# Fillers at chunk 3, a bank-wise wait, norms, turns and folds placed anew, and outputs stored by tile

## The chip, the cores and the metric

The kernel runs on one core of one Trainium2 chip. The metric is the device time of one execution in microseconds; lower is better. Before the change the median of three runs is 759.34 us (758.0 to 760.5).

## The reference

Three blocks follow each other on 4 batches of 768 tokens. In NumPy, cut to what is computed:

```python
# 1. gated linear attention, 8 heads of 48, q k v alpha: (4, 8, 768, 48)
for t in range(S):
    state = alpha[:, :, t, :, None] * state + einsum('bhd,bhe->bhde', k[:, :, t], v[:, :, t])
    y[:, :, t] = einsum('bhd,bhde->bhe', q[:, :, t], state)
x = y by token: (4, 768, 384)
# 2. spatial gating
h = gelu_tanh(x @ w_in); u, v = halves of h            # w_in: 384 x 1024
v_n = (v - mean) / sqrt(var + 1e-6) * g_ln
v_s = einsum('ts,bsd->btd', w_sg, v_n) + b_sg          # w_sg: 768 x 768
x = x + (u * v_s) @ w_out                              # w_out: 512 x 384
# 3. Fourier mixing and a two-layer network
u = x + real(fft(fft(x, axis=1), axis=2))
un = (u - mean) / sqrt(var + 1e-6)
return u + maximum(un @ w_ch1, 0) @ w_ch2              # 384 x 1536, 1536 x 384
```

## The kernel before

Every fp32 product of blocks 2 and 3 is made of three passes over operands split into a high and a low fp32r part (`product`, L1115). ScalarE copies the high part (x_hi, gated_hi, hidden_hi, ut_hi, fold_hi, w_c_hi), and VectorE subtracts it to get the low part. So nearly every step of TensorE waits for a copy on ScalarE and a subtraction on VectorE. Each engine runs its steps in order, and the orders are lists written out by hand.

**The first batch's attention** is worked in six chunks of 128 tokens by `FIRST_PE`, `FIRST_DVE` and `FIRST_ACT`. VectorE's step "query" makes qu (qu_b for odd chunks), TensorE's step "scores" first transposes the decayed keys (L1136), then multiplies them with qu (L1146). `keep_warm` (L1121) issues small products on constants into a free bank; `WARM_SCORES` and `WARM_OUT` say at which chunks, how many.

**Phase 1** (block 2, and the next batch's attention beside it) runs once for each batch by `P1_ORDER`: products v0 to v5 and u0 to u7, each followed by a gelu on ScalarE, then s0 to s7, the spatial products with w_sg. s_i writes bank i % 2; u3 used bank 0 and u4 bank 1 before it. Behind the product of s_i come the output products o_(i-1) with w_out (L1115 too), and o7 at ("end", 0). VectorE and ScalarE make gated, gated_hi and gated_lo of each s_i; `add_x` adds the residual (x1_half), POOL copies two columns, and SP stores x1 to DRAM (x_scratch).

In the last batch's phase 1 the Fourier mixing of batch 0 is worked in: `LAST_P1_AT` lists, by the step they follow, fold 0 to 3 (VectorE), folded 0 and 1 (fold_hi and fold_lo), z 0 to 3 and nyquist (TensorE and copies), mix, stats, norm 0 to 5 (VectorE), turn 0 to 5 (TensorE transposes a normed tile, L1320) and turned 0 to 5 (ut_hi on ScalarE, ut_lo on VectorE). "split n" splits weight piece n of the second network; "split hi" and "split lo" are its halves. SP loads the pieces 6 to 11 as their buffers come free: piece 9 when s7 is done (s_done), 10 when gated 7 is done, 11 when o7 is done (po_done).

**Phase 2** (block 3) has 26 slots for a batch. Slot k holds h_k (hidden tile k: TensorE, relu on ScalarE, hidden_lo on VectorE), then o_(k-2) (output products into three accumulators), and then what a table says: `P2_FIRST_AT` for batch 0, `P2_AT` for the others, mixing the next batch. "left" steps are those of batch 0's own mixing that phase 1 left over. "keep" copies u into ub on ScalarE and waits for the last x1 store, since ub lies over x1's tile. h_k waits for hidden_lo k-2, o_k for hidden_lo k. "fin" adds the accumulators to ub after o11 and o23, and SP stores each tile. A fold reads x_quarters, of which SP loads half and POOL the other half by indirect DMA, with `kept` at 2 and turn 5 done as the condition for batch 1; u_new, the residual, is loaded by both queues in the same way.

## Time and profile before

| what | value |
|---|---|
| median of 3 runs | 759.34 us |
| profiled execution | 764.03 us |
| its span, first to last instruction | 762.2 us |
| TensorE, VectorE, ScalarE, POOL busy | 740.7, 460.4, 194.7, 74.6 us |
| mean granted TensorE clock | 0.983 |
| bytes moved by DMA | 54.04 MB |

Times in the rows are microseconds from the start of the span. PE is TensorE, PEld its weight load, DVE VectorE, ACT ScalarE, and SPq the DMA issues of SyncE. A bracket at the end of a timeline row is the idle time of that engine before the instruction, and what ended it. A granted clock of 1.00 is 2.4 GHz, 0.50 is 1.2 GHz.

### The profile page before, as it was taken

What the parts mean: (1) busy time and instruction counts of PE and PEld (TensorE: products, weight loads), DVE (VectorE), ACT (ScalarE), POOL (GpSimd) and SP (SyncE); (2) the same over time, 40 slices, a digit from 0 to 9 for tenths busy, and PEclk for the clock granted to TensorE, in tenths of its full rate; (3) what the DMA queues carried; (4) which work ended last, traced back from release to release, by engine and by line L of the source; (5) the groups of instructions that cost most, each with busy time, mean ns of one, the idle gap of its engine ahead of it and who ended that gap; (6) DMA issues with size and microseconds to landing.
All of it is one profiled execution on the core that took longest, in us unless ns stands there. A gap on an engine that the chain in (4) does not pass through costs nothing.

```text
span 762.2 us, 11949 instructions
## 1 busy us (share of the span) xinstructions
PE 740.7 (97%) x4824; PEld 717.4 (94%) x4824; DVE 460.4 (60%) x872; ACT 194.7 (26%) x366; POOL 74.6 (10%) x122
## 2 busy tenths in 40 slices
PE   8999999999999999999998889999999999999997
PEld 7889999999999999988998879999999999999997
DVE  7979858797666966668588455445353735432221
ACT  1236111242112411134314322213211332122111
POOL 1013000030000300042110302001210010000000
PEclk9799999999999999999999989999999999999999
DMA  9623132231321313062315402002120020000000
GB/s 294 180 56 121 48 94 79 79 94 47 95 79 42 84 48 94 32 187 85 105 57 171 136 1 85 21 32 63 37 68 1 31 62 31 0 31 1 1 32 31
DMA packets 21000, 54.04 MB, mean 71 GB/s; under 512 B 2356, under 2 KB 14776, under 8 KB 20952
## 3 DMA queue, kind: packets, MB, share of 16 engines
q1 hardware_dynamic: 18104, 44.53, 19.3%
q0 software_dynamic: 2704, 8.71, 3.9%
q8 instruction: 34, 0.56, 0.3%
q10 hardware_dynamic: 144, 0.13, 0.1%
q14 instruction: 14, 0.11, 0.1%
HBM read 43.90 MB, written 9.46 MB: 70 GB/s over the span
## 4 chain that ended last, share of the span: by engine, by line
PE 88%; DVE 6%; issue 2%; ACT 2%; DMA 1%; POOL 1%; DVEq 0%; SPq 0%
PE bank L1115 72%; PE bank L1173 5%; PE bank L1146 3%; PE bank L1169 3%; PE bank L1161 2%; PE bank L1204 1%; PE bank L1136 1%; PE bank L1320 1%; DVE u_kept L1075 1%; DMA x_quarters<-x_scratch,mirrored_rows 1%; DMA decay_k_q<-in_akq 1%; DVE fold_f_sin L988 0%; POOL x_quarters L623 0%; ACT vn_hi L707 0%; ACT w_c_hi L694 0%
## 5 line engine op out<-in xcount | busy, mean ns | idle before, releaser
L1115 PE MATMUL bank<-ut_hi,w_c 128*128 128x384 f32 x576 | 164.7, 341 | 1.9 <-DVE hidden_lo L1066 1.9
L1066 DVE SCALAR_TENSOR_TENSOR hidden_lo<-bank,hidden_hi 128x384 fp32r<-128x384 f32 x96 | 53.4, 556 | 126.9 <-ACT hidden_hi L795 125.5
L1115 PEld LDWEIGHTS bank<-ut_hi,w_c 128*128 128x128 f32 x576 | 106.3, 189 | 2.3 <-DVE hidden_lo L1066 2.3
L795 ACT ACTIVATE hidden_hi<-bank 128x384 fp32r<-128x384 f32 x96 | 47.3, 492 | 205.4 <-PE bank L1115 205.4
L1115 PE MATMUL bank<-w_c_hi,hidden_hi 128*128 128x384 f32 x288 | 96.7, 336 | 0.7 <-DVE u_kept L1075 0.7
L1115 PE MATMUL bank<-ut_lo,w_c 128*128 128x384 f32 x288 | 96.9, 336 | 0.0
L1115 PE MATMUL bank<-w_c_hi,hidden_lo 128*128 128x384 f32 x288 | 96.3, 334 | 0.0
L1115 PE MATMUL bank<-w_c_lo,hidden_hi 128*128 128x384 f32 x288 | 96.2, 334 | 0.0
L1115 PE MATMUL bank<-w_sg_hi,vn_hi 128*128 128x384 f32 x192 | 67.6, 352 | 1.8 <-ACT u_gelu L728 1.8
L1115 PE MATMUL bank<-w_sg_lo,vn_hi 128*128 128x384 f32 x192 | 65.2, 340 | 0.0
L1115 PE MATMUL bank<-w_sg_hi,vn_lo 128*128 128x384 f32 x192 | 65.1, 339 | 0.0
L1115 PEld LDWEIGHTS bank<-w_c_hi,hidden_hi 128*128 128x128 f32 x288 | 54.2, 188 | 1.9 <-issue 1.9
L1115 PEld LDWEIGHTS bank<-ut_lo,w_c 128*128 128x128 f32 x288 | 54.6, 190 | 0.0
L1115 PEld LDWEIGHTS bank<-w_c_lo,hidden_hi 128*128 128x128 f32 x288 | 54.2, 188 | 0.0
L1115 PEld LDWEIGHTS bank<-w_c_hi,hidden_lo 128*128 128x128 f32 x288 | 54.1, 188 | 0.0
L749 ACT CAST gated_hi<-gated 128x384 fp32r<-128x384 f32 x32 | 16.4, 512 | 141.6 <-DVE gated L973 141.6
L1115 PEld LDWEIGHTS bank<-w_sg_hi,vn_hi 128*128 128x128 f32 x192 | 36.8, 192 | 3.5 <-issue 2.4
L1173 PE MATMUL bank<-values,sm 128*128 128x48 f32 x288 | 39.9, 266 | 0.0
L969 DVE SCALAR_TENSOR_TENSOR gated<-bank,g_col,bias_sg 128x384 f32<-128x384 f32 x32 | 19.7, 615 | 30.3 <-PE bank L1115 30.2
L1173 PEld LDWEIGHTS bank<-values,sm 128*128 128x128 f32 x288 | 37.2, 192 | 0.0
L889 DVE TENSOR_TENSOR sm<-bank,constants 128x512 f32<-128x512 f32 x42 | 27.0, 685 | 16.7 <-PE bank L1146 16.7
L1115 PEld LDWEIGHTS bank<-w_sg_lo,vn_hi 128*128 128x128 f32 x192 | 37.0, 193 | 0.0
(191 smaller groups left out, 1466.7 us busy)
## 6 DMA issues: line engine op xcount, KB each, us to landing
decay_k_q<-in_akq SPq DMA_DIRECT2D x19, 673.8 KB, 5.3
x_scratch<-x_half SPq DMA_DIRECT2D x8, 579.0 KB, 3.9
out_tiles<-u_kept SPq DMA_DIRECT2D x24, 192.0 KB, 2.0
values<-in_v SPq DMA_DIRECT2D x18, 192.0 KB, 5.1
x_quarters<-x_scratch SPq DMA_DIRECT2D x16, 168.9 KB, 3.4
raw_first_a<-in_w_first SPq DMA_DIRECT2D x3, 768.0 KB, 4.4
raw_first_b<-in_w_first SPq DMA_DIRECT2D x3, 768.0 KB, 4.7
raw_weights_b<-in_w_second SPq DMA_DIRECT2D x3, 768.0 KB, 4.3
```

The source lines that it names most:

```text
L749: nc.scalar.copy(gs[0][:, i % 3, :], gt[:, i % 3, :]).then_inc(ghi_done, 1)
L795: nc.scalar.activation(hid[0][:, i % 4, :], HB[i % 2][:, 0:HS], ACT.Relu).then_inc(hhi_done, 1)
L889: nc.vector.tensor_tensor(sm[:, :, x, :], sc[x][:].rearrange("p (a t) -> p a t", a=4), mask[:].unsqueeze(1).to_broadcast([P, 4, P]), ALU.m ...
L969: nc.vector.scalar_tensor_tensor(out=gt[:, i % 3, :], in0=GB[i % 2][:, 0:HS], scalar=g_col[:, f:f + 1], in1=bias_sg[:, h * HS:(h + 1) * HS ...
L1066: nc.vector.scalar_tensor_tensor(out=hid[1][:, i % 4, :], in0=HB[i % 2][:, 0:HS], scalar=0.0, in1=f32(hid[0][:, i % 4, :]), op0=ALU.max, o ...
L1075: nc.vector.tensor_tensor(ub[:, HT * i + j, :], ACC[j][:, 0:DM], ub[:, HT * i + j, :], ALU.add).then_inc(fin_done, 1)
L1115: ins = nc.tensor.matmul(dst, a, c, start=start and n == 0, stop=stop and n == len(passes) - 1)
L1136: ins = nc.tensor.transpose(ky[:, g * PR:(g + 1) * PR], kd[:, g, :], ident[0:PR, 0:PR])
L1146: ins = nc.tensor.matmul(sc[j][:, g * P:(g + 1) * P], kd[at, g, :], qu[at, g, :], start=True, stop=True)
L1161: ins = nc.tensor.matmul(sc[0][0:PR, g * PP:(g + 1) * PP], kn[:, g, :], values[:, g * PP:(g + 1) * PP], start=True, stop=True)
L1169: nc.tensor.matmul(ky[:, g * PP:(g + 1) * PP], qu[:, g, :], std[:, c % 2, g, :], start=True, stop=False, skip_group_check=True)
L1173: ins = nc.tensor.matmul(ky[:, h * D:(h + 1) * D], sm[:, g, j, :], values[:, h * D:(h + 1) * D], start=c == 0, stop=True, skip_group_check ...
```

## The change

- `WARM_SCORES` gets five filler products at chunk 3's scores.
- In phase 1, s0 waits for the gelu of u3 and s1 for that of u4 (in place of all eight at s0); o0 waits for all eight. In batch 0 the old wait stays.
- In the last phase 1, "folded 0" moves from behind u5 to behind u7. A new place, "product of s" 7, lies between s7's product and what follows it; turn 2 and turned 2 move there. Norm 3 moves up behind s6, turn 3 and norms 4 and 5 behind s7, turns 4 and 5 to the end of the phase. The split of piece 8 stands whole behind s7, and the high half of piece 9 at the end of the phase.
- In the first phase 2 only turned 3, 4 and 5 are left over. keep 0 and keep 1 both stand in slot 2. The folds move from slots 5 to 7 to slots 6 to 9, z from 8 to 10 to 10 to 12, mix 0 from 10 to 13, and the steps behind it by one to three slots. Pieces 9, 10 and 11 are split at h0, h3 and h4 (before: h0, h1, h3).
- SP loads piece 11 ahead of the last x1 store, and waits for POOL's quarters of batch 1 before it loads that batch's residual.
- In the last batch, o22 and o23 are worked together, accumulator by accumulator, with a semaphore of their own, and the last additions wait for it tile by tile.

```diff
 
 
-WARM_EARLY, WARM_SCORES, WARM_OUT = 8, {0: 3}, {0: 5, 1: 4}
+WARM_EARLY, WARM_SCORES, WARM_OUT = 8, {0: 3, 3: 5}, {0: 5, 1: 4}
 
...
          19: [("turn", 2), ("turned", 1), ("norm", 3)], 20: [("turned", 2), ("turn", 3), ("norm", 4)],
          21: [("turn", 4), ("norm", 5)], 22: [("turn", 5)], 24: [("turned", 3), ("turned", 4)], 25: [("turned", 5)]}
-P2_FIRST_AT = {0: [("left", ("turn", 3)), ("left", ("norm", 4)), ("left", ("turned", 3))],
-               1: [("left", ("turn", 4)), ("left", ("norm", 5)), ("left", ("turned", 4))],
-               2: [("left", ("turn", 5)), ("left", ("turned", 5)), ("keep", 0)], 3: [("keep", 1)],
-               5: [("fold", 0)], 6: [("fold", 1), ("fold", 2)], 7: [("fold", 3), ("folded", 0)],
-               8: [("folded", 1), ("z", 0)], 9: [("z", 1), ("z", 2)], 10: [("z", 3), ("nyquist", 0), ("mix", 0)]}
+P2_FIRST_AT = {1: [("left", ("turned", 3)), ("left", ("turned", 4))], 2: [("left", ("turned", 5)), ("keep", 0), ("keep", 1)],
+               6: [("fold", 0)], 7: [("fold", 1)], 8: [("fold", 2)], 9: [("fold", 3), ("folded", 0)],
+               10: [("folded", 1), ("z", 0)], 11: [("z", 1), ("z", 2)], 12: [("z", 3), ("nyquist", 0)], 13: [("mix", 0)],
+               14: [("stats", 0)], 15: [("mix", 1)], 16: [("stats", 1), ("mix", 2)], 17: [("stats", 2)],
+               18: [("norm", 0)], 19: [("turn", 0), ("norm", 1)], 20: [("turn", 1), ("turned", 0), ("norm", 2)],
+               21: [("turn", 2), ("turned", 1), ("norm", 3)], 22: [("turned", 2), ("turn", 3), ("norm", 4)],
+               23: [("turn", 4), ("norm", 5)], 24: [("turn", 5), ("turned", 3), ("turned", 4)], 25: [("turned", 5)]}
 
...
 
 P2_ORDER = phase2_order(P2_AT)
-P2_FIRST = phase2_order({k: P2_FIRST_AT.get(k, [] if k < 11 else P2_AT.get(k, [])) for k in range(2 * NF + LAG)})
+P2_FIRST = phase2_order(P2_FIRST_AT)
 FOURIER_STEPS = ("fold", "folded", "z", "nyquist", "mix", "stats", "norm", "turn", "turned")
-SPLIT_IN_P2 = {0: 9, 1: 10, 3: 11}
+SPLIT_IN_P2 = {0: ("split lo", 9), 3: ("split", 10), 4: ("split", 11)}
 
 
 LAST_P1_AT = {("v", 5): [("fold", 0)], ("u", 3): [("fold", 1), ("fold", 2)], ("u", 4): [("fold", 3)],
-              ("u", 5): [("folded", 0)], ("s", 0): [("folded", 1), ("z", 0), ("z", 1), ("split", 6)],
+              ("u", 7): [("folded", 0)], ("s", 0): [("folded", 1), ("z", 0), ("z", 1), ("split", 6)],
               ("s", 1): [("z", 2), ("z", 3), ("nyquist", 0)], ("s", 2): [("split", 7), ("mix", 0), ("stats", 0)],
               ("s", 3): [("mix", 1), ("stats", 1)], ("s", 4): [("mix", 2)],
               ("s", 5): [("stats", 2), ("norm", 0), ("norm", 1)],
-              ("s", 6): [("turn", 0), ("turn", 1), ("turned", 0), ("norm", 2), ("turned", 1), ("split hi", 8)],
-              ("s", 7): [("turn", 2), ("turned", 2), ("split lo", 8)], ("end", 0): [("norm", 3)]}
+              ("s", 6): [("turn", 0), ("turn", 1), ("turned", 0), ("norm", 2), ("turned", 1), ("norm", 3)],
+              ("product of s", 7): [("turn", 2), ("turned", 2)],
+              ("s", 7): [("turn", 3), ("norm", 4), ("norm", 5), ("split", 8)],
+              ("end", 0): [("turn", 4), ("turn", 5), ("split hi", 9)]}
 
...
         hlo_done = sem("hlo_done")
         o_done = sem("o_done")
+        o_tile_done = sem("o_tile_done")
         fin_done = sem("fin_done")
...
                     sp.wait_ge(z_done, 4)
                 need(sp, kept, 2 * m)
+                if m == 1:
+                    sp.wait_ge(quarters_in[1], 128)
                 sp.dma_start(ua[:, 0:HT, 0:DM], x1_dram[m][0:HS, 0:DM].rearrange("(j p) n -> p j n", p=P)).then_inc(
...
             sp.wait_ge(gt_done, 8 * B)
             load_piece(sp, NP1 + KD + 1)
-            store_x1(B - 1, "end", 0)
             sp.wait_ge(po_done, 8 * B)
             load_piece(sp, NP1 + KD + 2)
+            store_x1(B - 1, "end", 0)
             load_quarters(1)
...
                             vn_hi(b, NT - 4 + i)
                     elif step == "s":
+                        if isinstance(b, int) and b == B - 1:
+                            beside_last_phase1("product of s", i)
                         act.wait_ge(gt_done, 8 * b + i + 1)
...
                         need(act, o_done, k - 3)
                         nc.scalar.activation(hid[0][:, i % 4, :], HB[i % 2][:, 0:HS], ACT.Relu).then_inc(hhi_done, 1)
-                        if i in SPLIT_IN_P2 and isinstance(b, int) and b == 0:
-                            split_hi(SPLIT_IN_P2[i])
+                        if i in SPLIT_IN_P2 and isinstance(b, int) and b == 0 and SPLIT_IN_P2[i][0] == "split":
+                            split_hi(SPLIT_IN_P2[i][1])
 
...
                         nc.vector.tensor_tensor(gt[:, i % 3, :], gt[:, i % 3, :], ug[:, f, h * HS:(h + 1) * HS],
                                                 ALU.mult).then_inc(gt_done, 1)
+                        if isinstance(b, int) and b == B - 1:
+                            beside_last_phase1("product of s", i)
                         gated_lo(b, i)
...
                                                        op1=ALU.subtract).then_inc(hlo_done, 1)
                         if i in SPLIT_IN_P2 and isinstance(b, int) and b == 0:
-                            split_lo(SPLIT_IN_P2[i])
+                            split_lo(SPLIT_IN_P2[i][1])
                     elif step == "fin":
                         dve.wait_ge(kept, 2 * b + i + 1)
-                        dve.wait_ge(o_done, 2 * NF * b + NF * (i + 1))
+                        last = isinstance(b, int) and b == B - 1 and i == 1
+                        if not last:
+                            dve.wait_ge(o_done, 2 * NF * b + NF * (i + 1))
                         for j in range(HT):
+                            if last:
+                                dve.wait_ge(o_tile_done, j + 1)
                             nc.vector.tensor_tensor(ub[:, HT * i + j, :], ACC[j][:, 0:DM], ub[:, HT * i + j, :],
...
                             if i == 0:
                                 pe.wait_ge(vlo_done, NT * (b + 1))
-                                pe.wait_ge(ug_done, 8 * (b + 1))
                                 if isinstance(b, int) and b == 0:
+                                    pe.wait_ge(ug_done, 8)
                                     pe.wait_ge(w_lo_done, NP1)
+                            if i < 2:
+                                pe.wait_ge(ug_done, 8 * b + 4 + i)
                             if i >= 2:
...
                                       [w[:, t, h * HS:(h + 1) * HS] for w in w_sg]) for t in range(NT)]
                                     ).then_inc(s_done, 1)
+                            if isinstance(b, int) and b == B - 1:
+                                for what, n in LAST_P1_AT.get(("product of s", i), []):
+                                    mixing(0, what, n)
 
...
                             f = j % 4
                             pe.wait_ge(glo_done, 8 * b + j + 1)
+                            if j == 0:
+                                pe.wait_ge(ug_done, 8 * (b + 1))
                             if j == 4:
...
                         if f == 0:
                             need(pe, fin_done, NT * b + HT * h)
+                        if isinstance(b, int) and b == B - 1 and i >= 2 * NF - 2:
+                            if i == 2 * NF - 1:
+                                for j in range(HT):
+                                    product(ACC[j][:, 0:DM],
+                                            [([x[:, n % 4, j * P:(j + 1) * P] for x in hid],
+                                              [w[:, n % NF, :] for w in w_c2]) for n in (i - 1, i)],
+                                            start=False).then_inc(o_tile_done, 1)
+                            continue
                         for j in range(HT):
```

## Rows read from the trace of the kernel before

**Rows 1.** The page of the profile: TensorE's line of the busy times

```profile
PE 740.7 (97%) x4824; PEld 717.4 (94%) x4824; DVE 460.4 (60%) x872; ACT 194.7 (26%) x366; POOL 74.6 (10%) x122
```

**Rows 2.** Waits of TensorE: us in total, times, longest us

```profile
PE bank L1115 <- DVE fold_lo L1001: 3.5, 1, 3.5
PE bank L1115 <- ACT u_gelu L728: 2.0, 2, 1.8
PE bank L1320 <- DVE u_norm_early L1048: 2.0, 2, 1.5
PE bank L1115 <- DVE hidden_lo L1066: 1.9, 1, 1.9
PE bank L1146 <- DVE qu_b L875: 1.8, 1, 1.8
...
PE bank L1115 <- DVE gated_lo L915: 0.7, 1, 0.7
...
PE bank L1115 <- DVE z_lo L1007: 0.6, 1, 0.6
```

**Rows 3.** Windows: length, busy PE, PEld, DVE, ACT, POOL, granted clock, DMA, GB/s

```profile
26.85:36.95 10.10, 10.10 (x44) 9.44 (x44) 9.94 (x15) 1.44 (x3) 0.00 (x0) 0.50 0.49 158
...
108.60:111.95 3.35, 3.35 (x22) 3.12 (x21) 1.29 (x2) 0.36 (x1) 0.00 (x0) 0.50 0.80 229
361.20:364.55 3.35, 3.35 (x13) 3.35 (x12) 0.00 (x0) 0.00 (x0) 0.00 (x0) 0.50 0.02 5
443.25:449.85 6.60, 5.32 (x22) 5.32 (x23) 3.12 (x5) 1.42 (x3) 0.00 (x0) 0.50 0.00 0
```

**Rows 4.** Timeline around chunk 3: start us, us, engine, line, instruction, idle before

```profile
9.95 1.38 PE L1121 MATMUL bank<-constants 128*128 128x128 f32 x10
...
24.48 0.69 DVE L875 TENSOR_TENSOR qu_b<-decay_k_q_d,fwd_b 112x512 f32<-112x512 f32 x1
...
37.21 0.69 DVE L875 TENSOR_TENSOR qu<-decay_k_q,fwd 112x512 f32<-112x512 f32 x1
...
41.62 1.16 PE L1146 MATMUL bank<-qu,kd 48*128 48x128 f32 x16
```

**Rows 5.** Timeline ahead of the last batch's first spatial product

```profile
353.24 1.46 DVE L910 TENSOR_TENSOR vn_lo<-v_gelu,vn_hi 128x512 fp32r<-128x512 f32 x2
...
358.35 0.83 ACT L757 CAST fold_hi<-fold_f_cos 97x772 fp32r<-97x772 f32 x1 [2.69 <-DVE fold_f_cos L997]
...
359.09 0.87 ACT L728 ACTIVATE u_gelu<-bank 128x384 f32<-128x384 f32 x2
```

**Rows 6.** Timeline at the seam, then two of the DMA issue rows (landing last)

```profile
404.49 0.55 DVE L1053 TENSOR_TENSOR ut_lo<-bank,ut_hi 128x384 fp32r<-128x384 f32 x1
...
405.97 0.34 SPq L480 DMA_DIRECT2D raw_weights_a<-in_w_second  x1
...
412.50 0.38 SPq L499 DMA_DIRECT2D x_scratch<-x_half  x1
...
x_scratch<-x_half SPq DMA_DIRECT2D x8, 579.0 KB, 3.9
...
raw_weights_a<-in_w_second SPq DMA_DIRECT2D x1, 768.0 KB, 4.2
```

**Rows 7.** Timeline of the quarters, a weight split and the first fold

```profile
423.58 1.76 DVE L839 TENSOR_TENSOR w_c_lo<-raw_weights_d,w_c_hi 128x1536 fp32r<-128x1536 f32 x1 [0.81 <-ACT w_c_hi L694]
...
424.88 1.35 POOL L623 DMA_INDIRECT x_quarters<-x_scratch,mirrored_rows  x1 [12.41 <-ACT u_kept L789]
...
429.01 0.92 POOL L623 DMA_INDIRECT x_quarters<-x_scratch,mirrored_rows  x1 [0.30 <-issue]
...
435.35 1.77 DVE L988 TENSOR_TENSOR fold_f_cos<-x_quarters 97x1544 f32<-97x1544 f32 x1 [6.33 <-DMA x_quarters<-x_scratch,mirrored_rows]
```

**Rows 8.** Timeline at the end of the kernel

```profile
754.02 0.56 DVE L1066 SCALAR_TENSOR_TENSOR hidden_lo<-bank,hidden_hi 128x384 fp32r<-128x384 f32 x1 [2.56 <-ACT hidden_hi L795]
...
758.25 1.49 DVE L1075 TENSOR_TENSOR u_kept<-bank,u_kept 128x384 f32<-128x384 f32 x3 [3.67 <-PE bank L1115]
```

## Prediction

> **What bounds the kernel now.** I read the page first: TensorE is busy for 740.7 of 762.2 us [rows 1], so an edit pays only where it removes one of TensorE's few waits or stretches at the half clock, and the whole of what can be had is small. The waits of TensorE come next [rows 2]: 3.5 us for a fold, 2.0 for u_gelu, 2.0 for two normed tiles, 1.9 for hidden_lo, 1.8 for qu_b, 0.7 for gated_lo, 0.6 for z_lo. They lie in three places (chunk 3 of the first batch, the start of the last spatial products, the seam of the two phases with what follows it). Then the windows in which the granted clock is 0.50, that is 1.2 and not 2.4 GHz [rows 3]: 10.1 us behind the wait for qu_b, 3.4 us from 108.6, 3.4 us behind the wait for u_gelu, and 6.6 us that begin inside the wait for the fold. A wait thus costs itself and, in three of the four long ones, half of a stretch behind it. The timeline around each place gives who is late [rows 4 to 8].
>
> **Fillers at chunk 3.** Five filler products are 10 instructions, 1.2 to 1.4 us as the 1.38 us of the same ten at 9.95 [rows 4]. They stand where TensorE waits 1.76 us for qu_b (ready at 25.17), so they cost nothing as long as they are shorter than that wait; at the half clock they would take 2.4 to 2.8 us and cost up to 1.0. About 0.5 us of idle stays. If the clock holds, the 10.1 us at 1.2 GHz shrink to some 5. VectorE doesn't follow: it is busy for 9.94 of these 10.10 us [rows 3] and finishes chunk 4's queries at 37.90 whatever TensorE does [rows 4]. Chunk 4's scores, which began at 41.62, can't begin before. Gain 41.6 - 38.0 = 3.6 us, not 5. Behind that point TensorE is full and VectorE had its own waits on TensorE, so both move up together. Bounds: 0 (the clock falls all the same) to 3.6. I take 3.6.
>
> **Bank-wise wait.** s0 now asks for u3's gelu, s1 for u4's, and only the first output product for all eight; in addition ScalarE copies the first fold behind u7 and not behind u5. Before, that copy at 358.35 held the last two gelus until 359.96 [rows 5]. What s0 needs else is v_lo, done at 354.70 [rows 5]. So s0 starts at once: 1.8 us of wait (2.0 in two waits, this the longest) [rows 2] and half of the 3.4 us behind it [rows 3] go, 3.5 together. The product after s0 is z0, which waits for folded_lo; VectorE ends that at about 361.1 and s0 takes 3.1 us (18 products; 9 are half a slot of 3.12, the 0.56 + 2.56 of [rows 8]) and ends at 361.2. That is the thinnest cover here: if it fails, 0.3 us.
>
> **Turns and norms at the seam.** Turns 3, 4 and 5 go from phase 2 to the end of phase 1. Norm 3 can follow turned 1, whose ut_lo ends at 405.04 [rows 6], so turn 3 is no longer behind three x1 additions (1.5 us, as the three of [rows 8]) and a weight split of 1.76 [rows 7]. I count from the end of s7 at 405.8, just before SP's issue at 405.97 that waits for it [rows 6]: turn 2 0.3, o6 1.56, turn 3 0.3, a wait for gated_lo of 0.4 (0.7 before, since ScalarE now copies gated 7 without the weight split ahead of it), o7, two turns 0.6, h0, h1, h2, o0 at 1.56 each: 416.8, where before the same work ended at 419.8. The waits gone are 2.0 for the two norms [rows 2] + 0.3 = 2.3 us; I take these and leave the rest. What is late next is piece 9, split at h0: issued at 405.97 and 4.2 us to landing [rows 6], copied by ScalarE until about 412.0, its low half by VectorE until 414.9, while o0 wants it at 415.2. One us more of landing costs 0.7. Bounds 1.0 to 3.0.
>
> **What the moved DMAs change.** On SP's queue the last x1 store goes behind piece 11, which waits for po_done: the store leaves at about 412.9, as before (412.50), but has 768 KB ahead of it. ScalarE's two keep copies wait for it, and both now stand in slot 2, ahead of the relu of h3. At 3.9 us to landing [rows 6] it is there at 416.8, and piece 11 beside it may make it 418.5. TensorE first misses that relu at h5, at 423.0; so the store may be 2 us later still before it costs anything. kept then reaches 2 near 419.8 against 424.6, and the quarter loads start 4.8 us earlier. On SP the residual of batch 1 now waits for POOL's quarters; behind it in that queue stands only the first half's output store, due some 40 us later.
>
> **Folds later.** The first fold waited 6.33 us for quarters, which landed 5.4 us after the last POOL issue had ended [rows 7], with the residual's 576 KB in the same engines. It held hidden_lo (1.9 us), then z0 waited 3.5 us for the fold, and the clock fell. Now the issues end near 425 and the quarters land by 430.4 at the same 5.4 us, sooner with the residual held back (427 to 431); the fold is asked for at 428.7 (slot 6 starts at 426.1, its h takes 1.56 and relu and hidden_lo the next 1.0), in slot 6, and the first product that would miss hidden_lo 7 is h9 at 435.4: a fold that starts by 433 is free. z0 comes in slot 10, behind one fold operation per slot (1.76 to 1.84 us of VectorE in 3.12). Gain 1.9 + 3.5, and half of the 5.32 us that TensorE worked in the slow window from 443.25 [rows 3], 2.7: 8.1. The product behind z3 is now in the next slot, 0.6 more. Bounds 4 (the landing as late as before in absolute time, a third of the stall and one slow stretch back) to 8.7.
>
> Here a rule speaks against the change. The first POOL issue took 1.35 us, the later ones 0.92, and it overlapped a weight split of 1.76 us, which ended at 425.34, by 0.46 [rows 7]. By the Trainium skill ("SBUF — State Buffer", Who interferes with whom) a VectorE instruction with two SBUF inputs blocks GpSimd's SBUF reads for its whole length; the rows agree (0.43 longer). Two splits of 1.76 us now run beside these POOL issues. By the rule they put the landing at 431 to 432 instead of 428, still inside the cover.
>
> **Output by tile.** The last two output steps run tile by tile. Three additions (1.49 us, 0.47 apart) followed the last product [rows 8]; now one does. Gain 0.95. Skipping o22 takes away what stood before o23, but hidden_lo 23 ends at 754.58 [rows 8] and o21 about 755.0, two half slots before the last product's end, so no wait comes.
>
> **Sum.** 3.6 + 3.5 + 2.3 + 8.1 + 0.6 + 0.95 = 19.1 us. The profiled execution took 764.03 us (span 762.2 and 1.8 around it), the median of the runs is 759.34, so 4.7 less. Taken from the profiled time the sum gives 744.9, from the median 740.2. Part of the 4.7 may be slow stretches that the change removes anyway. I take the middle, **742.5**.
>
> **The rivals.** (1) The fillers don't hold the clock, because the products behind them are small: in the window from 108.6 the clock fell after an idle time of only 0.7 us. Then 3.6 is missing: 746. (2) Quarters, store or piece 9 land late and a new stall at slots 2 to 7 takes the place of the fold's: 3 to 5 us back, 746 to 749. For it: the DMA engines are full around these transfers; against: covers of 2 and 4 us. (3) The edits do nothing that a run shows, since each freed wait is given back to VectorE, 60% busy over all but nearly full at chunk 3 and at the seam: 758. Against: it waits for TensorE in between. (4) Slower: ScalarE stands at keep 0 until the x1 store behind piece 11 lands; each us past 420.5 stalls TensorE from h5 on one for one, and moves kept and the quarters. It decides from the 19 us that the rest gains: only a landing 29 us after the issue makes 762. The landing of these stores is 3.9 us [rows 6], so little speaks for it.
>
> **How the numbers follow.** Forecast 0.64, rival 1 0.15, rival 2 0.14, rival 3 0.04, rival 4 0.03. The range runs from 740.2 less the 1.7 us that the slow window from 108.6 costs (it may shift away), 738.5, to rival 2's 749. About 0.3%, 2.3 us, is what a measurement of this kernel can tell from no change. Faster 0.94 (the forecast, rivals 1 and 2, and a quarter of rival 3), same 0.03 (the rest of rival 3), slower 0.03 (rival 4).
>
> **What would show it.** In the profile of the changed kernel: ten filler instructions before chunk 3's scores and a granted clock of 1.00 from 27 to 37; chunk 4's scores at 38; no wait for u_gelu before the last batch's s0; turns 3 to 5 ahead of h0, o0 without a wait; the first fold not waiting for quarters or less than 4 us; no window at 0.50 in phase 2; one addition behind the last product. A busy time of TensorE near 732 (740.7 less the halves of three slow stretches, plus the fillers) and a span near 743 would be right. Wrong would be a granted clock of 0.50 behind the fillers, or a wait of TensorE for hidden_lo in slots 4 to 9.

## The result and the profile after

The changed kernel takes 741.49 us (median of 4 runs, 741.35 to 743.57); the kernel before, run beside it, 759.92 us (4 runs, 758.0 to 763.5). The ratio is 0.976, 95% interval 0.972 to 0.980: 18.4 us less, between the medians. The profiled execution took 741.35 us; the one of before was one of the slowest of its kernel, so the two traces stand 22.7 us apart, and what follows says which of the two differences is meant.

The page of the profile after: span, busy times, the row of the granted clock over 40 slices.

```profile
span 739.5 us, 11977 instructions
...
PE 730.5 (99%) x4834; PEld 709.3 (96%) x4834; DVE 460.0 (62%) x872; ACT 194.5 (26%) x366; POOL 76.8 (10%) x122
...
PEclk9999999999999999999999999999999999999999
```

TensorE is busy for 730.5 us, where [rows 1] had 740.7, and its clock is at 2.4 GHz in every slice. The waits of TensorE after (us in total, times, longest):

```profile
PE bank L1141 <- DVE state_decayed L1093: 1.7, 1, 1.7
PE bank L1130 <- DVE w_in_lo L848: 0.9, 1, 0.9
PE bank L1151 <- ACT y_by_token_odd L710: 0.7, 1, 0.7
PE bank L1161 <- DVE qu_b L884: 0.6, 1, 0.6
...
PE bank L1130 <- DVE gated_lo L924: 0.2, 1, 0.2
```

Of the seven waits of [rows 2] the ones for the fold, u_gelu, the norms, hidden_lo and z_lo are gone; qu_b fell from 1.8 to 0.6 and gated_lo from 0.7 to 0.2. One is new: the wait for w_in_lo behind chunk 3, which the trace of before, with TensorE at half clock there, does not have. The windows after that answer to [rows 3] (length, busy PE, PEld, DVE, ACT, POOL, granted clock, DMA, GB/s):

```profile
24.00:37.00 13.00, 11.49 (x100) 10.56 (x100) 12.73 (x21) 3.84 (x5) 0.00 (x0) 1.00 0.50 152
100.00:110.00 10.00, 9.34 (x77) 8.98 (x76) 6.23 (x11) 1.08 (x3) 0.00 (x0) 1.00 0.33 89
352.00:362.00 10.00, 10.00 (x70) 9.81 (x69) 7.53 (x13) 4.74 (x7) 0.00 (x0) 1.00 0.08 33
430.00:450.00 20.00, 20.00 (x147) 19.92 (x146) 9.19 (x16) 5.14 (x11) 3.71 (x4) 1.00 0.16 39
```

All four are at 1.00. In the first VectorE is busy for 12.73 of 13.00 us while TensorE now has 1.5 us of idle: the bound there has passed to VectorE.

TensorE's timeline of after, at four places: the fillers with the scores of chunk 3 and of chunk 4; the first product of s0; the turns of the seam; the last product.

```profile
23.03 1.29 PE L1136 MATMUL bank<-constants 128*128 128x128 f32 x10
24.95 1.16 PE L1161 MATMUL bank<-qu_b,kd_b 48*128 48x128 f32 x16 [0.63 <-DVE qu_b L884]
...
37.68 1.16 PE L1161 MATMUL bank<-qu,kd 48*128 48x128 f32 x16
...
352.62 0.33 PE L1130 MATMUL bank<-w_sg_hi,vn_hi 128*128 128x384 f32 x1
...
396.80 0.49 PE L1342 MATMUL bank<-constants,u_norm_early 128*128 128x128 f32 x3
...
398.69 0.49 PE L1342 MATMUL bank<-constants,u_norm_early 128*128 128x128 f32 x3
399.40 0.45 PE L1130 MATMUL bank<-w_out_hi,gated_hi 128*128 128x384 f32 x1 [0.22 <-DVE gated_lo L924]
...
401.08 0.82 PE L1342 MATMUL bank<-constants,u_norm_early 128*128 128x128 f32 x6
...
736.22 0.34 PE L1130 MATMUL bank<-w_c_hi,hidden_lo 128*128 128x384 f32 x1
```

Chunk 4's scores begin at 37.68, where [rows 4] had 41.62. The place 352.62 of s0 was 360.10 before, and the end of s7, 396.80, was 405.8: 3.9, 7.5 and 9.0 us earlier. TensorE's last product, at 757.80 before, starts at 736.22, 21.6 us earlier, and the span is 22.7 us shorter. Over the whole span TensorE is idle for 21.5 us before (762.2 - 740.7) and for 9.0 after (739.5 - 730.5).

What carries the fold at the start of phase 2, from the timelines of SP, ScalarE, POOL and VectorE of after, one engine behind the other:

```profile
403.60 0.38 SPq L504 DMA_DIRECT2D x_scratch<-x_half  x1
...
409.31 2.21 ACT L798 COPY u_kept<-u_new_early 128x1152 f32<-128x1152 f32 x2 [1.81 <-DMA x_scratch<-x_half]
...
411.80 1.02 POOL L630 DMA_INDIRECT x_quarters<-x_scratch,mirrored_rows  x1 [8.23 <-ACT u_kept L798]
413.12 0.93 POOL L630 DMA_INDIRECT x_quarters<-x_scratch,mirrored_rows  x1 [0.31 <-issue]
414.36 1.50 POOL L630 DMA_INDIRECT x_quarters<-x_scratch,mirrored_rows  x1 [0.31 <-issue]
416.17 1.82 POOL L630 DMA_INDIRECT x_quarters<-x_scratch,mirrored_rows  x1 [0.30 <-issue]
...
413.31 1.76 DVE L848 TENSOR_TENSOR w_c_lo<-raw_weights_c,w_c_hi 128x1536 fp32r<-128x1536 f32 x1 [0.81 <-ACT w_c_hi L701]
...
415.45 1.75 DVE L848 TENSOR_TENSOR w_c_lo<-raw_weights_d,w_c_hi 128x1536 fp32r<-128x1536 f32 x1
...
420.15 1.77 DVE L999 TENSOR_TENSOR fold_f_cos<-x_quarters 97x1544 f32<-97x1544 f32 x1
```

The fold, which had waited 6.33 us for the quarters [rows 7], has no bracket: they are there when slot 6 asks, though with nothing to spare, since SP, which waits for POOL's quarters now, issues the residual at 420.13. The keep copies do wait, 1.81 us, for the store issued at 403.60, but TensorE doesn't follow.

### The profile page after: what moved, and what is told of

Its sections match the earlier page's. It is cut to its first block, busy times and chain, and to the rows that moved or that the text cites. A ratio compares the mean times of both kernels' runs of the same rounds, so it can differ in the third digit from the quotient of the medians.

```text
span 739.5 us, 11977 instructions
## 1 busy us (share of the span) xinstructions
PE 730.5 (99%) x4834; PEld 709.3 (96%) x4834; DVE 460.0 (62%) x872; ACT 194.5 (26%) x366; POOL 76.8 (10%) x122
## 4 chain that ended last, share of the span: by engine, by line
PE 94%; DVE 4%; issue 1%; DMA 1%; ACT 0%; SPq 0%; DVEq 0%
PE bank L1130 79%; PE bank L1188 5%; PE bank L1161 3%; PE bank L1184 2%; PE bank L1176 2%; PE bank L1151 1%; PE bank L1342 1%; PE bank L1219 1%; DVE u_kept L1090 1%; DMA decay_k_q<-in_akq 1%; DVE fwd_b L880 0%; DVE fwd L880 0%; DVE rev_b L868 0%; DVE w_in_lo L848 0%; DVE sm L898 0%
## 5 line engine op out<-in xcount | busy, mean ns | idle before, releaser
L1130 PE MATMUL bank<-ut_hi,w_c 128*128 128x384 f32 x576 | 162.8, 339 | 0.0
L1130 PEld LDWEIGHTS bank<-w_sg_hi,vn_lo 128*128 128x128 f32 x192 | 36.0, 188 | 0.0
```

The costliest lines, as they stand in the source:

```text
L1130: ins = nc.tensor.matmul(dst, a, c, start=start and n == 0, stop=stop and n == len(passes) - 1)
```

## The experiments

Each kernel was timed beside the kernel before on the same chip. Before ran 48 times in these comparisons: 756.2 to 765.1 us, with a mean granted clock of 0.983 to 0.995, never 1.000. They were taken in three groups, each on a chip of its own. That spread decides what single edits can show, so it comes first. Before's runs by clock (mean time, runs): 0.983: 764.0 (12); 0.984: 764.5 (4); 0.986: 762.3 (4); 0.988: 760.8 (7); 0.990: 759.3 (7); 0.992: 757.9 (4); 0.993: 757.8 (1); 0.995: 757.4 (9). A straight line through all 48 is, rounded, time = 753.9 us + 600 us x (1 - clock), and the runs scatter about it by 0.8 us. A clock of 0.983 is 25.8 us at 1.2 GHz in 760, so a microsecond of half clock costs about 0.4 us of time. With this line each run can be read at full clock (its time less 600 x (1 - clock)), which takes out of the comparison how the clock happened to fall. The mean of each kernel so read, with twice its standard error:

| kernel | runs | median us | mean clock | read at full clock |
|---|---|---|---|---|
| before | 48 | 760.2, 760.2, 761.3 in the three groups | 0.988 | 753.9 ± 0.2 |
| before + fillers | 10 | 758.71 | 0.993 | 754.3 ± 0.6 |
| before + tile outputs | 10 | 762.46 | 0.987 | 753.6 ± 0.2 |
| before + bank-wise wait | 10 | 757.75 | 0.991 | 751.7 ± 0.5 |
| before + later folds | 9 | 754.13 | 0.991 | 747.7 ± 0.8 |
| after with the old seam | 4 | 744.66 | 0.999 | 744.5 ± 0.3 |
| after with the old fold slots | 4 | 746.81 | 0.998 | 745.7 ± 0.6 |
| after without the fillers | 4 | 742.11 | 0.997 | 741.4 ± 0.3 |
| after | 4 | 741.49 | 0.999 | 741.5 ± 0.6 |

The slope is that of before; for kernels at a clock of 0.999 it hardly matters. For before it does: none of its runs is above 0.995, so its 753.9 is an extrapolation, and its groups do not lie exactly on the line (0.5 us above it at 0.995, 0.8 below at 0.992, 1.0 above at 0.984). The ± in the table is the scatter alone; differences between the kernels of before and those of after can be off by about 1 us more, an estimate from these distances.

**The fillers, added alone and taken out alone.** To before:

```diff
-WARM_EARLY, WARM_SCORES, WARM_OUT = 8, {0: 3}, {0: 5, 1: 4}
+WARM_EARLY, WARM_SCORES, WARM_OUT = 8, {0: 3, 3: 5}, {0: 5, 1: 4}
```

> The kernel before with the five filler products at chunk 3's scores and nothing else. Theory (the wait for qu_b lets the clock fall, the fillers hold it, and VectorE limits what that gives): granted clock 1.00 from 27 to 37 us, chunk 4's scores near 37.7 in place of 41.62, and 3.6 to 3.9 us less, 755.5 to 756.5; if the window at the half clock near 108 goes with it, 1.7 more. Rival (the products behind the fillers are too small to hold the clock): a window at 0.50 between 27 and 37 stays, gain under 1.5 us. Rival (the gain is the full half of the 10.1 us): 5 us less.

Measured: 758.71 us (757.38 to 760.29), ratio 0.9964, interval 0.9933 to 0.9994. Windows of its profiled execution:

```profile
26.85:36.95 10.10, 9.45 (x78) 8.49 (x74) 9.94 (x16) 2.02 (x4) 0.00 (x0) 1.00 0.58 181
108.00:115.00 7.00, 7.00 (x54) 7.00 (x54) 4.38 (x8) 0.60 (x2) 1.21 (x1) 1.00 0.21 55
356.50:360.00 3.50, 3.50 (x13) 3.50 (x12) 0.18 (x1) 0.00 (x0) 0.00 (x0) 0.51 0.02 5
441.00:446.00 5.00, 5.00 (x25) 5.00 (x24) 1.78 (x3) 1.00 (x2) 0.00 (x0) 0.66 0.01 3
```

The stretch that stood at 0.50 in [rows 3] is at 1.00; the one near 108 is gone too, and the ones of u_gelu and of the fold remain. The median moved by 1.4 us against the group's 760.15 and the mean by 2.0 (758.74 against 760.79), short of the 3.6 expected. The other way round, after with `3: 5` taken out:

> The changed kernel without the fillers at chunk 3. Theory: the half clock from 27 to 37 us comes back and with it 3.6 to 3.9 us, 745 to 745.5. If the slow window near 108 was tied to the shift of the schedule by the fillers, it comes back too: 747. Rival (the clock fell in the profile of before by chance of its phase): no change in most runs, 741.5.

Measured: 742.11 us (741.46 to 748.14), ratio 0.9755, interval 0.9682 to 0.9827: not to be told from after, as the rival had it. Two of the four runs have a clock of 1.000 without any filler (741.46 and 741.59), one has 0.988 (748.14). In the profiled one (742.62, clock 0.998) the wait for qu_b is 1.8 us again and the clock falls only briefly:

```profile
25.00:30.00 5.00, 4.23 (x31) 4.01 (x32) 4.46 (x7) 2.81 (x3) 0.00 (x0) 0.66 0.46 122
30.00:36.00 6.00, 6.00 (x47) 5.50 (x46) 5.88 (x10) 0.86 (x2) 0.00 (x0) 1.00 0.80 258
```

What the stretch costs can be read without the jitter of the start, as the distance from chunk 3's scores to chunk 4's. It is 12.73 us after (24.95 to 37.68) and in before + fillers (25.97 to 38.70); 16.39 in before (25.23 to 41.62) and in before + bank-wise wait (25.38 to 41.77), both with the clock down for about 10 us; 13.29 in after without fillers (25.77 to 39.06), with the clock down for 3.4 us. And it is 12.72 in before + later folds, which has no fillers and waited 1.76 us like before, but kept its clock. Its timeline, and then its window:

```profile
25.30 1.16 PE L1150 MATMUL bank<-qu_b,kd_b 48*128 48x128 f32 x16 [1.76 <-DVE qu_b L879]
...
38.02 1.16 PE L1150 MATMUL bank<-qu,kd 48*128 48x128 f32 x16
```

```profile
26.00:38.00 12.00, 11.12 (x96) 10.23 (x92) 11.81 (x18) 2.48 (x5) 0.00 (x0) 1.00 0.41 135
```

So the price of 3.66 us is right where the clock falls, but the fall behind this wait is not certain. Same wait and same work behind it gave about 10 us of half clock, 3.4 us, or none. Over all the profiled executions: without fillers at chunk 3 the clock falls there in four of five, with two or five fillers in none of nine.

**Fewer fillers, and fillers at a second place.** After with two products instead of five, and after with two more ahead of the wait for y_by_token_odd in the first piece of phase 1:

```diff
-WARM_EARLY, WARM_SCORES, WARM_OUT = 8, {0: 3, 3: 5}, {0: 5, 1: 4}
+WARM_EARLY, WARM_SCORES, WARM_OUT = 8, {0: 3, 3: 2}, {0: 5, 1: 4}
```

> The changed kernel with two fillers at chunk 3's scores and not five, so about 1.3 of 1.76 us of wait stay idle. Theory (the clock falls with the share of idle time, by chance of phase, and without fillers two of four runs fell): some runs of ten show a clock of 0.995 or less and take 744 to 748, the fastest 741.4 and the median 741.5 to 743. Rival (any work in the gap is enough): as the changed kernel with five.

```diff
+                    if not before and isinstance(n, int) and n == 1 and c == 3:
+                        keep_warm(sc[1], 2)
                     need(pe, yn_done, i - before)
```

> The changed kernel with two more filler products in the first phase 1, at batch 1's chunk 3, where TensorE waits 0.66 us for y_by_token_odd. They are 4 instructions, 0.5 us, inside that wait. Theory (what is left of the spread between the runs of the changed kernel, 741.4 to 745.6, is a stretch at half clock behind such small waits, by chance of phase): the fastest runs stay at 741.4, fewer runs show a clock under 0.999, and the median falls by 0 to 0.5 us. Rival (the rest of the spread comes from another place): the same spread as the changed kernel, 741.4 to 745.6.

Measured: 741.50 us (741.47 to 742.07, 6 runs) with two, 741.34 us (741.17 to 742.24, 6 runs) with a second place. All twelve runs have a clock of 1.000. With two products it is held although 1.3 us of the wait for qu_b stay, as the rival had it. The second place is 0.15 us under after, less than either kernel's own spread, so it is not shown to be a gain: with two products and no second place the six clocks are 1.000 as well.

**The bank-wise wait alone**, in before, with the copy of the fold behind u7 as in the change:

```diff
-              ("u", 5): [("folded", 0)],
+              ("u", 7): [("folded", 0)],
...
-                                pe.wait_ge(ug_done, 8 * (b + 1))
                                 if isinstance(b, int) and b == 0:
+                                    pe.wait_ge(ug_done, 8)
                                     pe.wait_ge(w_lo_done, NP1)
+                            if i < 2:
+                                pe.wait_ge(ug_done, 8 * b + 4 + i)
```

> The kernel before with the bank-wise waits of s0, s1 and o0 and the first folded step moved behind u7, nothing else. Theory: the 1.8 us wait for u_gelu ahead of the last batch's s0 goes and so does the 3.4 us at half clock behind it: 3.5 us less, 756. Rival (z0 or VectorE waits instead): the wait goes but under 1.5 us are won.

Measured: 757.75 us (752.25 to 760.05, 10 runs), ratio 0.9933, interval 0.9896 to 0.997. The wait of 1.8 us for u_gelu is gone from its list (one of 0.2 is left) and the clock is 1.00 behind it:

```profile
27.00:38.00 11.00, 11.00 (x50) 10.16 (x49) 10.81 (x16) 1.44 (x3) 0.00 (x0) 0.53 0.48 149
352.00:362.00 10.00, 10.00 (x69) 9.81 (x68) 8.94 (x13) 3.91 (x8) 0.00 (x0) 1.00 0.25 80
```

At full clock it stands 2.2 us under before; 1.8 was the wait. The median moved by 2.4 us and the mean by 3.9, where 3.5 was expected. One of its runs, at a clock of 1.000, took 752.25. In that profile TensorE's wait for the fold is 1.9 us, not 3.5, with the clock down around it (433 to 437, 440 to 444). TensorE, at half clock ahead of the wait, came to it about 1.7 us later, half of the 3.4, and so waited 1.6 us less: that stretch cost next to nothing.

**The copy of the fold, put back** behind u5 in after:

```diff
-              ("u", 7): [("folded", 0)],
+              ("u", 5): [("folded", 0)],
```

> The changed kernel with the first folded step back behind u5, the bank-wise waits kept. Theory (the waits of s0 and s1 need only u3 and u4, whose gelus come before that copy): s0 still starts at once; only o0 needs all eight gelus, 3 us later: no change, 741.5. Rival (the move of the copy was what freed s0): the wait ahead of s0 and a stretch at half clock come back, 743.5 to 745.

Measured: 743.78 us (741.57 to 745.64, 4 runs); the runs above 745 have a clock of 0.995, those at 0.999 and 1.000 took 741.57 and 742.35. In the profiled one (741.57) no wait for u_gelu stands ahead of s0. The bank-wise wait alone does it. Read at full clock the kernel stands at 742.0 ± 0.7, after at 741.5 ± 0.6; whether the copy's place has a part in the two lower clocks, four runs don't say.

**The folds: the later slots alone, and everything but them.** To before, from slot 6 on the table of after (slots 0 to 3 as before); and after with before's slots 5 to 10:

```diff
-               5: [("fold", 0)], 6: [("fold", 1), ("fold", 2)], 7: [("fold", 3), ("folded", 0)],
-               8: [("folded", 1), ("z", 0)], 9: [("z", 1), ("z", 2)], 10: [("z", 3), ("nyquist", 0), ("mix", 0)]}
+               6: [("fold", 0)], 7: [("fold", 1)], 8: [("fold", 2)], 9: [("fold", 3), ("folded", 0)],
+               10: [("folded", 1), ("z", 0)], 11: [("z", 1), ("z", 2)], 12: [("z", 3), ("nyquist", 0)], 13: [("mix", 0)],
...
```

> The kernel before with the folds, z, nyquist and mix of the first phase 2 in the later slots (folds 6 to 9, z 10 to 12, mix 0 at 13), nothing else; turns, keeps and DMA order as before. The quarters should land at 435.3 as before, the fold is asked for at 431.6, and the first product that misses hidden_lo 7 is h9 at 438.4. Theory (the slots give most of the cover): VectorE waits 3.7 in place of 6.3 us, TensorE waits for neither hidden_lo nor the fold at z0: 5.4 us of waits less and the window at half clock behind them gone in the profile, time 752 to 755. Rival (only the earlier quarters make the cover): TensorE still waits 2 us or more there, 757 or more.

> The changed kernel with the folds, z, nyquist and mix of the first phase 2 in the slots of before (folds 5 to 7, z 8 to 10), keeps, turns and DMA order as changed. Theory (both the earlier quarters and the later folds are needed): the quarters are in by 418 to 420, the fold is asked for at 416.5, so VectorE stands 2 to 3 us, folds in two slots of 3.12 us delay z0 by 1 to 3 us; 743 to 746 and perhaps one stretch at half clock. Rival (the earlier quarters alone did it): within 0.7 us of 741.5.

Measured: the slots alone 754.13 us (749.59 to 755.86, 9 runs), ratio 0.9899, interval 0.9865 to 0.9933; after without them 746.81 us (745.93 to 749.17, 4 runs), ratio 0.9836. In the first no wait for hidden_lo or z_lo is left, and one of 0.2 us for fold_lo, although the fold still waits 3.43 us for its quarters. In the second the quarters come at 420.8 and not at 435.3, but the fold is asked for earlier too and waits 2.50 us for them; TensorE waits 3.0 us for fold_lo and, as before, 0.6 for z_lo. The fold of the first; then VectorE from the step ahead of the fold to the low part that z0 needs, in the second; then TensorE's wait there:

```profile
430.43 1.77 DVE L992 TENSOR_TENSOR fold_f_cos<-x_quarters 97x1544 f32<-97x1544 f32 x1 [3.43 <-DMA x_quarters<-x_scratch,mirrored_rows]
```

```profile
417.75 0.55 DVE L1074 SCALAR_TENSOR_TENSOR hidden_lo<-bank,hidden_hi 128x384 fp32r<-128x384 f32 x1
420.80 1.77 DVE L996 TENSOR_TENSOR fold_f_cos<-x_quarters 97x1544 f32<-97x1544 f32 x1 [2.50 <-DMA x_quarters<-x_scratch,mirrored_rows]
...
428.96 0.95 DVE L1009 TENSOR_TENSOR fold_lo<-fold_f_cos,fold_hi 97x772 fp32r<-97x772 f32 x1
```

```profile
PE bank L1127 <- DVE fold_lo L1009: 3.0, 1, 3.0
```

The slots are worth 6.2 us on before and 4.2 us on after, both at full clock, where 743 to 746 had been expected for the second kernel. The lesser gain on after is what the earlier quarters had taken already (no wait for hidden_lo, half a microsecond less for the fold). What is left in the second is mostly the quarters after all: VectorE was free at 418.30 and stood for 2.50 us, then worked without a pause from 420.80 to 429.91, and z0 had been due at 427.0. Had the quarters been there at 418.3, the same work would have ended about 427.4, an estimate from these rows, and about 0.5 of the 3.0 us would be left. So the later slots alone are enough, and quarters another 2.5 us earlier would have done nearly as much; that no run tried.

**What brings the quarters early, undone.** After without SP's new wait for the quarters ahead of the residual, and after with the x1 store ahead of piece 11 again:

```diff
-                if m == 1:
-                    sp.wait_ge(quarters_in[1], 128)
```

> The changed kernel without SP's wait for POOL's quarters ahead of the residual load of batch 1. Theory: the residual's 576 KB share the DMA engines with the quarters as before, these land 1 to 3 us later, at 420 to 423, and the first fold has cover until about 425: no change of the time, 741.5, but VectorE may wait for quarters by up to 2 us. Rival (the hold is what keeps TensorE from waiting): 1 us or more slower.

```diff
+            store_x1(B - 1, "end", 0)
             sp.wait_ge(po_done, 8 * B)
             load_piece(sp, NP1 + KD + 2)
-            store_x1(B - 1, "end", 0)
```

> The changed kernel with SP's last x1 store again ahead of piece 11. Theory: the store leaves at the same time (403.6) with less traffic ahead of it and lands 1 to 2 us earlier, ScalarE's 1.81 us wait at the first keep shrinks, and as TensorE had cover there the time is the same, 741.5. Rival (the order of store and piece decides the time of the quarters and with it the fold): 1 us or more either way.

Measured: 741.66 us (741.52 to 744.68, 4 runs) and 741.84 us (741.22 to 743.71, 4 runs). The fold of the first, then the keep copies of the second:

```profile
422.39 1.77 DVE L997 TENSOR_TENSOR fold_f_cos<-x_quarters 97x1544 f32<-97x1544 f32 x1 [1.93 <-DMA x_quarters<-x_scratch,mirrored_rows]
```

```profile
408.56 2.21 ACT L798 COPY u_kept<-u_new_early 128x1152 f32<-128x1152 f32 x2 [0.28 <-DMA x_scratch<-x_half]
```

Without the hold the quarters come some 2 us later and VectorE waits 1.93 us for them. With the store first the keep copies start 0.75 us earlier, though the store left 0.78 us later in that execution, so 1.5 us sooner after its issue. Neither reaches TensorE, and neither shows in the time of four runs, in these slots.

**The seam, put back**: turns 3 to 5, the norms, the weight splits and keep 1 where before has them, the rest as after.

```diff
-              ("product of s", 7): [("turn", 2), ("turned", 2)],
-              ("s", 7): [("turn", 3), ("norm", 4), ("norm", 5), ("split", 8)],
-              ("end", 0): [("turn", 4), ("turn", 5), ("split hi", 9)]}
+              ("s", 7): [("turn", 2), ("turned", 2), ("split lo", 8)], ("end", 0): [("norm", 3)]}
...
-SPLIT_IN_P2 = {0: ("split lo", 9), 3: ("split", 10), 4: ("split", 11)}
+SPLIT_IN_P2 = {0: ("split", 9), 1: ("split", 10), 3: ("split", 11)}
```

> The changed kernel with turns 3 to 5, norms 3 to 5, the split of pieces 8 to 11 and keep 1 placed as before; later folds, DMA order, fillers, bank-wise waits and tile outputs stay. Theory: the two waits for norms at h1 and h2 (0.5 and 1.5 us) and the longer wait for gated_lo come back, 2.3 us, and the quarters start later by as much again without touching the fold: 743.5 to 744.5. Rival (the later quarters take the cover of the fold): 746 or more with a wait of TensorE for hidden_lo near slot 6.

Measured: 744.66 us (744.13 to 747.38, 4 runs), ratio 0.9804, interval 0.9752 to 0.9855. Its waits:

```profile
PE bank L1342 <- DVE u_norm_early L1059: 2.0, 2, 1.5
...
PE bank L1130 <- DVE gated_lo L924: 0.7, 1, 0.7
```

Both stalls are back, and profile against profile, both at a clock of 1.000, it is 744.13 - 741.35 = 2.8 us, as expected (743.5 to 744.5), and no wait for hidden_lo appears.

**The outputs by tile alone**, in before: the change's own lines for o_tile_done.

```diff
+                            if last:
+                                dve.wait_ge(o_tile_done, j + 1)
...
+                        if isinstance(b, int) and b == B - 1 and i >= 2 * NF - 2:
+                            if i == 2 * NF - 1:
```

> The kernel before with o22 and o23 of the last batch worked together, accumulator by accumulator, and the last three additions waiting tile by tile, nothing else. Theory: one addition and not three behind the last product, 0.95 us less, 758.8 to 759. Rival (skipping o22 exposes hidden_lo 23, or the store of the last tile queues behind the others): 0 to 0.4 us less or a wait of TensorE ahead of the last step.

Measured: 762.46 us (757.26 to 764.01, 10 runs), ratio 1.0006, interval 0.9972 to 1.004. The median shows nothing of it: read at full clock it is 0.3 us under before, give or take 0.3, where 0.95 was expected. The trace shows it: from the start of TensorE's last product to the end of the span it is 3.3 us here (756.82 to 760.1), 4.4 in before (757.80 to 762.2), 3.3 after (736.22 to 739.5). The end of after on VectorE:

```profile
734.59 0.56 DVE L1090 TENSOR_TENSOR u_kept<-bank,u_kept 128x384 f32<-128x384 f32 x1 [1.62 <-PE bank L1130]
735.55 0.56 DVE L1090 TENSOR_TENSOR u_kept<-bank,u_kept 128x384 f32<-128x384 f32 x1 [0.41 <-PE bank L1130]
736.60 0.56 DVE L1090 TENSOR_TENSOR u_kept<-bank,u_kept 128x384 f32<-128x384 f32 x1 [0.49 <-PE bank L1130]
```

Two additions run while TensorE still multiplies; in [rows 8] all three came behind it.

## Why the prediction was right, step by step

The forecast of 742.5 us is 1.0 us above the 741.49 measured; the sum of 19.1 us stands against 18.4 between the medians. That it came so near is in part luck: the forecast is the middle between 744.9 (from the profiled time) and 740.2 (from the median), and the prediction chose the middle with one sentence and no working. It helps to split that sum into waits and clock. The waits in it are 1.8 (u_gelu) + 2.3 (seam) + 5.4 and 0.6 (folds, z_lo) + 0.95 (outputs) = 11.05 us; the clock is 3.6 + 1.7 + 2.7 = 8.0. Measured at full clock, before and after are 753.9 - 741.5 = 12.4 us apart. The single edits add up to that: bank-wise wait 2.2, later folds 6.2, seam 2.9, outputs 0.3 by the runs and 1.1 by the trace, together 11.6 to 12.4, and so do the two traces, with 21.5 - 9.0 = 12.5 us less idle time of TensorE. The rest, 18.4 - 12.4 = 6.0 us, is the clock. So the waits were sized 1.3 us too small and the clock 2.0 us too large, and the two errors partly cancel. The split is good to about 1 us, as said under the table.

**Fillers.** The mechanism holds: they fit in the wait, 0.63 us of idle stays (0.5 forecast), and chunk 4's scores follow VectorE, at 37.68 (38 forecast). The step that was too sure is that the 3.6 us are there in every execution. On before they were worth 1.4 us of the median and 2.0 of the mean, on after 0.6 of the median, since the fall they prevent is not certain. 3.6 is the price where the clock is down for about 10 us. It was the largest mis-sized term, and the trace of before, one execution at a clock of 0.983, could not show that it was an unfavourable one; the 4.7 us between that execution and the median could have been read as this sign.

**Bank-wise wait.** Right: s0 follows u7 without a gap and its window is at 1.00. The thin cover held: z0 begins at 355.80, in order behind s0, without a wait. That the copy of the fold had to move was not a needed step. Behind u5 it held nothing once s0 no longer asked for all eight gelus.

**Seam.** Right in place, a little small in size: 2.3 forecast, 2.8 to 2.9 measured. The prediction's own count of the steps gave 3.0 (416.8 against 419.8), and it left 0.7 of that out. The wait for gated_lo was put at 0.4 and is 0.2. Piece 9 was the step with the least cover, 0.3 us, and it held: the products h0, h1, h2 and o0 have no wait.

**Moved DMAs.** The first keep copy, which waits for the store, started 5.7 us after its issue (403.60 to 409.31); 3.9 to 5.6 was allowed for, and its cover was enough. The store left 9.3 us earlier than the forecast's 412.9, nearly all of it the 9.0 us by which s7 ends earlier: the prediction had counted in before's absolute times. The quarters were in time. The new waits and the new order, which the prediction weighed at length, make no difference to the time either way in the later slots; whether they would in the old ones no run shows.

**Folds.** 5.4 + 0.6 us of waits forecast, 6.2 measured. The reason it gave, covers of 2 and 4 us from earlier quarters and later slots together, was more than is needed. The slots alone remove all but 0.2 us of wait on before, where the quarters are as late as ever; the quarters as early as this change has them leave, without the slots, 3.0 us at z0, of which 2.5 are the first fold's wait for them. The 2.7 us of clock was short: from h6 to the next batch's h0 the two traces differ by 9.7 us, 6.2 of it idle time and 3.4 busy time, with 6.8 us at half clock in it before.

Here the rule on the shared port can be read too. The third issue starts at 414.36 inside the split that ends at 415.07 and lasts 1.50 us; the fourth starts at 416.17 inside the one that ends at 417.20 and lasts 1.82. The second started at 413.12, ahead of the split of 413.31, and took its 0.93 all the same; the split was not longer for it either (1.76 us, as ever). Each delayed issue ends 0.79 us after the VectorE instruction in which it began, as in [rows 7] (0.89). They cost 0.57 + 0.89 = 1.5 us in all. For POOL that agrees with the Trainium skill ("SBUF — State Buffer", Who interferes with whom), by which the engine that comes second waits until the instruction of the first is over; VectorE, where it came second, did not wait. The prediction had charged both splits in full, 3.5 us, where only what is left of one counts.

**Outputs by tile.** 0.95 forecast, 1.1 in the trace; too small for the medians.

**Rivals.** The fillers did hold the clock at chunk 3 (rival 1), in all nine profiled executions that have them. They don't rule out a fall elsewhere: of the 36 runs of after and its variants with fillers five show 0.995 and take 3.2 to 4.1 us more than the fastest of their kernel. None of the five was profiled, so where the clock fell in them stays open. No new stall came at slots 2 to 7 (rival 2). The gains were not given back to VectorE (rival 3). Behind chunk 3 VectorE sets the pace, with a new wait of 0.9 us for w_in_lo, but the 3.6 had allowed for that. The store did not hold up the keep copies for long (rival 4): 1.81 us, and no wait of TensorE follows from it. Two sums of this part were off: 3 to 5 us back from 742.5 is 745.5 to 747.5, not rival 2's 746 to 749, from which the upper end of the range comes; and in rival 4, 762 is reached by a landing 27 us after the issue when counted from the forecast (7.6 of cover and 19.5), 29 only from 740.2. Neither touches the outcome.

TensorE's busy time was put at 732 and is 730.5; the slow window at 108.60, which the forecast left in, is gone from the trace of after, and it held 1.7 us. Its wait of 0.66 us for y_by_token_odd is still there. Profile against profile, 3.9 us are gained up to chunk 4's scores, 1.7 at 108, 1.8 ahead of s0, 1.5 behind it, 2.9 at the seam, 9.7 at the folds and 1.1 at the end, 22.6 of 22.7 us. The sum was made from the profiled execution's rows, and against this difference it is 3.6 us short: 1.7 left in at 108, 1.0 at the folds, 0.6 at the seam, 0.3 at chunk 3 and 0.1 at the end, less 0.2 around s0. Against the medians it is 0.7 too much, since most runs of before have less slow clock than that execution.

## What to carry to other kernels

Ahead of a sum, ask whether the profiled execution is a typical one. Its mean granted clock, set beside that of other runs, tells how much of the time is slow clock that may or may not come again; cost a wait at its own length, and what the clock adds behind it as a chance. Where an engine in order works off a chain of pieces and another waits for the last, compare when the chain starts, how long it is and when its end is due: later slots and earlier data are two ways to the same cover, and one of them may be enough. Before a guard on a DMA queue is counted on, look whether anybody waits at the end of it.

## What the runs showed of the hardware

- The clock's fall behind a short wait is not certain: what stands in the program does not decide it. After 1.76 us of idle and the same small products it fell for about 10 us in three kernels' profiled executions, for 3.4 us in a fourth, and not at all in a fifth; behind the 0.66 us at 104 to 108 it fell for 3.4 us in before, 6.8 us in before + tile outputs and in no other profile here. Over 48 runs of before this spreads one kernel's time by 8.9 us (756.2 to 765.1).
- The cost over runs of before is close to a straight line (within 1.0 us for the groups above): 600 us x (1 - mean clock), that is 0.4 us for each microsecond at 1.2 GHz, rather than the 0.5 of a TensorE that is never held by another engine. At chunk 3, 10 us cost 3.66 and 3.4 us cost 0.56; VectorE, busy for 9.94 of 10.10 us there [rows 3], sets the pace of the rest.
- With two filler products in a wait of 1.8 us the clock stayed at 1.000 in 6 runs of 6, with 1.3 us of idle left; with none in 2 runs of 4.
- An indirect DMA issue on POOL (0.93 us) that starts within one of VectorE's 1.76 us weight splits or folds, which have two inputs in SBUF, ends 0.8 to 0.9 us after that instruction; one that starts ahead of it is not delayed, and does not delay it.
